# A three-stage fp32 kernel on one core: sums of squares added by transfers, the last downward products of a tile placed behind the next tile's second pair

## The chip, the core and the metric

The kernel runs on one core of a Trainium2 chip. The metric is the time of one execution on the device, in microseconds (us); the median of three runs before the change is 1011.33 us.

## What is computed

```python
mag = np.sqrt(a_re * a_re + a_im * a_im)
scale = np.minimum(mag, 0.999) / (mag + 1e-06)
a_re_n, a_im_n = (a_re * scale, a_im * scale)
for t in range(S):                       # B, H, S, D = 4, 8, 768, 48
    ar, ai = (a_re_n[:, :, t, :, None], a_im_n[:, :, t, :, None])
    new_re = ar * S_re - ai * S_im
    new_im = ar * S_im + ai * S_re
    kv = np.einsum('bhd,bhe->bhde', k[:, :, t], v[:, :, t])
    S_re, S_im = (new_re + kv, new_im)
    y[:, :, t] = np.einsum('bhd,bhde->bhe', q[:, :, t], S_re)
# then, with x = y as (3072, 384):
h = x @ w_in                             # d_ff 2048
x = (np.maximum(h, 0.0) + np.log1p(np.exp(-np.abs(h)))) @ w_out
h = (x @ w1) * (x @ w2) @ w3             # d_ff 1024
out = h @ w_out2
```

## The kernel before, in words

The 3072 tokens are eight tiles of 384. A tile passes three stages. The **preparation** (ScalarE, VectorE) makes from `a_re`, `a_im`, `q`, `k` the decayed queries and keys: it normalizes a by its magnitude, multiplies the a of eight neighbouring tokens up (`run` 1 to 7), combines the ends of these runs (`ends`, `carry` 1 to 32), multiplies the carries in (`by`, `p`), makes `tt` = q p (`q`) and `pp` = k / p (`inverse`, `keys`, `keys end`). Two sums of squares stand in it, both of two halves of the tile `te`, 128 x 1152 each: |a|^2 (`m2`) ahead of the square root, and |p|^2 (`p2`) ahead of the reciprocal. ScalarE squares both halves, VectorE adds them (L928 and L1017), ScalarE takes the logarithm (L663 and L692) and exponentials, and VectorE refines with Newton steps (`newton`, `scale start`, `scale`, `a`; or `inverse`). `tt` and `pp` go to memory and come back with another layout (`stq`, `stk`).

The **attention** of a tile is six groups (`scores` L1317 and L1320, mask on VectorE L1119, `outputs` L1340 to L1349). ScalarE copies each group's y to `ys` (L721), and small transfers place it into `x1raw` (`store_y`, L416, eight per chunk of 128 tokens, issued by SyncE). The **first network** takes `x1raw` split in two halves of precision (`x1h`, `x1l`), in eight pairs of 128 columns: `up` (18 products into `ps_ay` for pair 0 and into `ps_p` for the others), the softplus on ScalarE (Abs L732, Exp L736, Ln L738) and VectorE (`add_relu`, L1165), the split `g_h` (ScalarE, L745) and `g_l` (VectorE, L1172), and `down` (18 products into `ps_2`). At the end of a tile `x2_out` (ScalarE, L787) copies `ps_2` over `x1raw`, which SyncE stores. The second network runs after the eighth tile.

The order is written out by hand for each engine, in a function `slot(n, ...)` of eight steps j. Slot n holds the first network of tile n, the attention of tile n + 1, the preparation of tile n + 2 and the first sum of tile n + 3. On TensorE step j is `up` of pair j + 1, the scores of group j, `down` of pair j, the outputs of group j. In step 6 `up` of the next tile's pair 0 follows, and step 7 is `down` of pair 7. On VectorE the dictionaries `before_mask`, `after_mask` and `after_sum` tell which pieces of the preparation stand where in a step. Each engine waits for semaphores in its own order: SyncE's transfers and ScalarE's and VectorE's instructions behind a wait stand still with it. `up` of a pair above 0 waits for the `add_relu` of the pair before it, the scores of group 0 for the `add_relu` of the running tile's pair 0, since both use `ps_ay`. GpSimd computes only in the second network (`ab_low`).

Before the first slot come the preparations of tiles 0 and 1 and the attention of tile 0, one after the other, while the weights are loaded and split.

## Time and profile before

| | |
|---|---|
| runs | 1012.21, 1008.62, 1011.33 us, median 1011.33 |
| profiled execution | 1010.65 us, span 1008.9 us |
| busy in the span | PE 912.0 us (90%), DVE 607.4 (60%), ACT 426.8 (42%), POOL 70.4 (7%) |
| mean granted TensorE clock | 0.959 |

PE is TensorE, PEld its weight loads, DVE VectorE, ACT ScalarE, POOL GpSimd, SP SyncE. A share of busy time is a mean over the start, the seven tile slots, and the second network; the stretches and waits of the section after the next tell them apart. "Idle before" is the time for which an engine stood still ahead of an instruction, with what released it. Neighbouring matmuls overlap, so the durations of the single ones add up to more than the time they take.

### The profile page before, as it was taken

The numbers are of one execution on the slowest core, as the hardware profiler recorded it, in microseconds if no ns is written. First come the engines' busy times: TensorE is split into PE (matmuls) and PEld (weight loads), VectorE is DVE, ScalarE is ACT, GpSimd is POOL, SyncE is SP. The second block draws the span as 40 slices with busy tenths as digits, with TensorE's granted clock in tenths as the row PEclk, the third lists the DMA queues.
The fourth block names the chain that finished last, engine by engine and source line by source line (L and its number), as shares of the span: only waits on it lengthen the run. The fifth ranks groups of instructions, "written<-read, shape, count | busy, mean of one in ns | idle before, by whom it ended". The sixth has DMA issues, their size and how long they took to land.

```text
span 1008.9 us, 14507 instructions
## 1 busy us (share of the span) xinstructions
PE 912.0 (90%) x5442; PEld 828.5 (82%) x5442; DVE 607.4 (60%) x966; ACT 426.8 (42%) x618; POOL 70.4 (7%) x56
## 2 busy tenths in 40 slices
PE   0964839999999999999989999987999999999998
PEld 0533739988999888989889999987888888888887
DVE  5977978989989989989899723445121212121211
ACT  3152254673764664853854654667011111212011
POOL 0000000000000000000000000000222222222221
PEclk9985569999999999999999999999999999999999
DMA  9676074381470570560650630232101010101000
GB/s 338 227 201 176 20 205 110 106 196 55 137 207 13 152 192 10 169 176 13 196 145 12 174 78 12 72 124 79 32 1 63 1 63 0 62 0 63 1 32 32
DMA packets 98663, 99.52 MB, mean 99 GB/s; under 512 B 6944, under 2 KB 91936, under 8 KB 98592
## 3 DMA queue, kind: packets, MB, share of 16 engines
q1 hardware_dynamic: 98592, 98.59, 34.1%
q8 instruction: 42, 0.69, 0.3%
q14 instruction: 29, 0.24, 0.1%
HBM read 63.96 MB, written 29.88 MB: 93 GB/s over the span
## 4 chain that ended last, share of the span: by engine, by line
PE 47%; DVE 28%; DVEq 9%; ACT 8%; issue 4%; DMA 3%; ACTq 1%; SPq 0%
PE ps_p L1281 5%; PE ps_p L1282 5%; PE ps_p L1283 5%; DVE sp L1165 4%; DVEq L921 3%; PE ps L1469 3%; PE ps L1467 3%; PE ps L1468 3%; DVE g_l L1172 2%; DVE am L1119 2%; PE ps L1281 2%; PE ps L1283 2%; PE ps L1282 2%; PE ps_ay L1317 2%; DVE an L953 2%
## 5 line engine op out<-in xcount | busy, mean ns | idle before, releaser
L1281 PE MATMUL ps<-g_h,wo_h 128*128 128x384 f32 x384 | 133.5, 348 | 7.1 <-DVE g_l L1172 7.1
L629 POOL TENSOR_TENSOR abl<-ab,abh 128x512 fp32r<-128x512 f32 x48 | 69.5, 1447 | 931.7 <-DVE abh L1263 931.7
L1281 PE MATMUL ps_p<-x1h,win_h 128*128 128x384 f32 x336 | 117.3, 349 | 15.7 <-DVE sp L1165 15.3
L1283 PE MATMUL ps<-g_h,wo_l 128*128 128x384 f32 x384 | 129.4, 337 | 0.0
L1282 PE MATMUL ps<-g_l,wo_h 128*128 128x384 f32 x384 | 129.1, 336 | 0.0
L1283 PE MATMUL ps_p<-x1h,win_l 128*128 128x384 f32 x336 | 113.1, 337 | 0.0
L1282 PE MATMUL ps_p<-x1l,win_h 128*128 128x384 f32 x336 | 113.0, 336 | 0.0
L745 ACT ACTIVATE g_h<-sp 128x768 fp32r<-128x768 f32 (+1 forms) x71 | 55.5, 781 | 98.2 <-DVE sp L1165 98.2
L1317 PE MATMUL ps_ay<-stq,stk 96*128 96x128 f32 x384 | 57.5, 298 | 34.7 <-DMA vt<-in_v 13.3
L1254 DVE TENSOR_TENSOR ab<-ps_ay,bc 128x512 f32<-128x512 f32 x24 | 16.6, 693 | 117.0 <-ACT bc L892 117.0
L1317 PEld LDWEIGHTS ps_ay<-stq,stk 96*128 96x128 f32 x384 | 54.9, 211 | 35.9 <-issue 23.4
L1254 DVE TENSOR_TENSOR ab<-ps_p,bc 128x512 f32<-128x512 f32 x24 | 16.6, 693 | 110.4 <-ACT bc L892 110.4
L732 ACT ACTIVATE sp<-ps_p 128x768 f32<-128x768 f32 (+1 forms) x63 | 46.3, 736 | 81.2 <-PE ps_p L1283 81.2
L1281 PEld LDWEIGHTS ps<-g_h,wo_h 128*128 128x128 f32 x384 | 72.7, 189 | 9.5 <-DVE g_l L1172 9.4
L1281 PEld LDWEIGHTS ps_p<-x1h,win_h 128*128 128x128 f32 x336 | 63.6, 189 | 19.7 <-DVE sp L1165 19.0
L1165 DVE SCALAR_TENSOR_TENSOR sp<-ps_p,sp 128x768 f32<-128x768 f32 (+1 forms) x63 | 54.6, 867 | 39.0 <-ACT sp L738 35.5
L1172 DVE TENSOR_TENSOR g_l<-sp,g_h 128x768 fp32r<-128x768 f32 (+1 forms) x71 | 62.3, 878 | 24.4 <-ACT g_h L745 19.0
L1282 PEld LDWEIGHTS ps<-g_l,wo_h 128*128 128x128 f32 x384 | 72.8, 190 | 0.0
L1283 PEld LDWEIGHTS ps<-g_h,wo_l 128*128 128x128 f32 x384 | 72.5, 189 | 0.0
L892 ACT ACTIVATE bc<-ps_p 128x512 f32<-128x512 f32 x24 | 14.4, 599 | 126.4 <-PE ps_p L1283 126.4
L892 ACT ACTIVATE bc<-ps_k 128x512 f32<-128x512 f32 x24 | 14.4, 599 | 126.0 <-PE ps_k L1283 126.0
L1282 PEld LDWEIGHTS ps_p<-x1l,win_h 128*128 128x128 f32 x336 | 63.7, 190 | 0.0
(147 smaller groups left out, 2053.4 us busy)
## 6 DMA issues: line engine op xcount, KB each, us to landing
qk_scr<-tt SPq DMA_DIRECT2D x16, 576.0 KB, 4.5
stq<-qk_scr SPq DMA_DIRECT2D x48, 192.0 KB, 4.8
qk_scr<-pp SPq DMA_DIRECT2D x16, 576.0 KB, 4.1
stk<-qk_scr SPq DMA_DIRECT2D x48, 192.0 KB, 4.6
an<-in_a_re SPq DMA_DIRECT2D x8, 576.0 KB, 4.1
an<-in_a_im SPq DMA_DIRECT2D x8, 576.0 KB, 5.2
qk<-in_q SPq DMA_DIRECT2D x8, 576.0 KB, 7.5
qk<-in_k SPq DMA_DIRECT2D x8, 576.0 KB, 8.7
```

The costliest lines, as they stand in the source:

```text
L629: tensor_tensor(abl[:, m % AR, :], ab[:, m % 2, :], abh[:, m % AR, :].bitcast(F32), ALU.subtract).then_inc(ab_lo, 1)
L732: act(buf, ps_u[j][:, us, 0:T], ACT.Abs)
L745: act(g_h[:, j % GR, us, :], sp[:, j % 2, us, :], ACT.Copy).then_inc(g_hi, us.stop - us.start)
L921: eng.drain()
L1165: ve.scalar_tensor_tensor(out=buf, in0=ps_u[j][:, us, 0:T], scalar=0.0, in1=buf, op0=ALU.max, op1=ALU.add)\
L1172: ve.tensor_tensor(g_l[:, j % GR, us, :], sp[:, j % 2, us, :], g_h[:, j % GR, us, :].bitcast(F32), ALU.subtract).then_inc(g_lo, us.stop - ...
L1254: ve.tensor_tensor(ab[:, m % 2, :], ps_ab[m % 2][0], bc[:, m % 2, :], ALU.mult).then_inc(ab_mul, 1)
L1281: mm(o, wh, xh, start=start, stop=False)
L1282: mm(o, wh, xl, start=False, stop=False)
L1283: return mm(o, wl, xh, start=False, stop=stop)
L1317: last = mm(ps_a[:, h4, :], stk[0:D2, h, cs], stq[0:D2, h, cs], start=True, stop=True)
L1467: mm(ps_o[s_], ah, w34h[:, m, :], start=m == 0, stop=False)
```

## The change

1. The two adds of squares leave VectorE. GpSimd issues a transfer from one half of `te` to the other that adds (`accum_op`), 16 in all, and ScalarE's logarithm waits for its landing.
2. The transfers of y (`store_y`) move from SyncE's queue to GpSimd's. There `sum_psquares` of a tile stands behind the y of group 3, and `sum_squares` behind that of group 4 and ahead of that of group 5.
3. On TensorE `down` of a tile's pair 7 moves behind `up` of the next tile's pair 1; each part of `down` of pair 0 waits for its own third of `x2_out`.
4. ScalarE: `x2_out` moves between Abs and the rest of pair 1's softplus; the logarithm of |a|^2 moves from ahead of `x1_high` to between Abs and Exp of pair 7; both squares of p come between Abs and Exp.
5. VectorE: `scale` moves ahead of `add_relu` of pair 0, and `a` is split in two, the first half ahead of `g_low`; `run` 7, `by` and later pieces are spread anew, `keys end` goes to step 6.

The diff, without the hunks that only pass a new argument and that on VectorE ahead of the first slot:

```diff
@@ -467,10 +460,6 @@
             wait(w34_ev, NM2)
             eng.dma_start(w34_scr.rearrange("c p n -> p c n"), w34s[:, :, :]).then_inc(w34_wr, 16)
             load_piece(7)
-
-            wait(raw_lo, 5)
-            for i in range(NG):
-                store_y(0, i)
             wait(prep_p, 4)
             load_a(2)
             store_q(1)
...
@@ -486,29 +475,17 @@
 
                 if not first:
                     store_x2(n - 1)
-                if att:
-
-                    if first:
-                        wait(x1_lo, 2)
-                    else:
-                        x2_landed(n - 1)
-                    for i in range(NG - 2):
-                        store_y(n + 1, i)
                 if prep:
                     wait(prep_p, 2 * n + 6)
                     if nxt:
                         load_a(n + 3)
                     store_q(n + 2)
-                if att:
-                    store_y(n + 1, NG - 2)
                 if prep:
 
                     wait(yz_mm, NG * n + NG + 4)
                     for c in range(2):
                         stack_q(n + 2, c)
                         load_v(n + 2, c)
-                if att:
-                    store_y(n + 1, NG - 1)
                 if prep:
                     store_k(n + 2)
                     for c in range(2):
...
@@ -629,6 +606,45 @@
                 tensor_tensor(abl[:, m % AR, :], ab[:, m % 2, :], abh[:, m % AR, :].bitcast(F32),
                               ALU.subtract).then_inc(ab_lo, 1)
 
+            def store_y(m, i):
+                c, hq = i // 2, i % 2
+                eng.wait_ge(y_ev, NG * m + i + 1)
+                for u, row, rows, pairs, p0, gs_ in Y_MOVES[hq]:
+                    eng.dma_start(x1raw[p0:p0 + rows, gs_, CT * c:CT * c + CT], ys[64 * u + row:64 * u + row + rows, i % 2, pairs, :])\
+                        .then_inc(y_wr[i], 16)
+
+
+            def sum_squares(m):
+                eng.wait_ge(prep_sq, m + 1)
+                eng.dma_start(te[:, 0, :], te[:, 1, :], accum_op=ALU.add).then_inc(prep_m2, 16)
+
+            def sum_psquares(m):
+                eng.wait_ge(prep_psq, m + 1)
+                eng.dma_start(te[:, 0, :], te[:, 1, :], accum_op=ALU.add).then_inc(prep_p2, 16)
+
+            sum_squares(0)
+            sum_psquares(0)
+            sum_squares(1)
+
+            eng.wait_ge(raw_lo, 5)
+            for i in range(NG):
+                store_y(0, i)
+            sum_psquares(1)
+            sum_squares(2)
+            for m in range(1, NT):
+
+                if m == 1:
+                    eng.wait_ge(x1_lo, 2)
+                else:
+                    for mo in range(G):
+                        eng.wait_ge(x2_wr[mo], 16 * m)
+                for i in range(NG):
+                    store_y(m, i)
+                    if m < NT - 1 and i == 3:
+                        sum_psquares(m + 1)
+                    if m < NT - 2 and i == 4:
+                        sum_squares(m + 2)
+
             with eng.Fori(0, NT2) as t:
                 for m in range(NM2):
                     ab_low(t, m)
...
@@ -659,7 +675,7 @@
                 last.then_inc(prep_sq, 1)
 
             def prep_log(m):
-                eng.wait_ge(prep_m2, m + 1)
+                eng.wait_ge(prep_m2, 16 * m + 16)
                 act(te[:, 1, :], te[:, 0, :], ACT.Ln)
 
             def prep_root(m):
...
@@ -730,7 +746,7 @@
                     buf = sp[:, j % 2, us, :]
                     eng.wait_ge(p_mm, after(n, j, us))
                     act(buf, ps_u[j][:, us, 0:T], ACT.Abs)
-                    if between is not None:
+                    if between is not None and us.start == 0:
                         between()
                     eng.drain()
                     act(buf, buf, ACT.Exp, scale=-1.0)
...
@@ -808,25 +824,27 @@
                     if j < NP1 - 2:
 
                         def between():
+                            if prev and j == 0:
+
+                                eng.wait_ge(x1_lo, 2 * n + 2)
+                                x2_out(n - 1)
                             if has_prep and j == 4:
-                                prep_psquare(n + 2, 0)
-                            k_by_tokens(n + 1, j)
-
-                        softplus(n, j + 1, split, between if att else None)
-                        if has_prep and j == 4:
-                            prep_psquare(n + 2, 1)
+                                prep_psquares(n + 2)
+                            if att:
+                                k_by_tokens(n + 1, j)
+
+                        softplus(n, j + 1, split, between)
                         if nxt_prep and j == 5:
                             prep_squares(n + 3)
                         g_high(n, j + 1, split)
                     elif j == NP1 - 2:
-                        if nxt_prep:
-                            prep_log(n + 3)
-                            prep_root(n + 3)
                         if nxt:
                             for part in range(2):
                                 y_loaded(n + 1, part)
                                 x1_high(n + 1, part)
-                        softplus(n, j + 1, split)
+                        softplus(n, j + 1, split, (lambda: prep_log(n + 3)) if nxt_prep else None)
+                        if nxt_prep:
+                            prep_root(n + 3)
                         g_high(n, j + 1, split)
                         if nxt_prep:
                             prep_root_square(n + 3)
...
@@ -837,13 +855,10 @@
                         w2_high(j)
                     elif weights and j == 2 * G:
                         w34_high()
-
-                if nxt:
-                    eng.wait_ge(x1_lo, 2 * n + 4)
-                if not weights:
+                if not nxt and not weights:
                     x2_out(n)
 
-            slot(0, True, True, True)
+            slot(0, True, True, True, prev=False)
             for n in range(1, NT - 3):
                 slot(n, True, True, True)
             slot(NT - 3, True, True, False)
...
@@ -924,9 +939,7 @@
                 eng.drain()
 
             def prep_m2_(m):
-                eng.wait_ge(prep_sq, m + 1)
-                ve.tensor_tensor(te[:, 0, :], te[:, 0, :], te[:, 1, :], ALU.add).then_inc(prep_m2, 1)
-                eng.drain()
+                pass
 
             def prep_newton(m):
 
...
@@ -949,9 +962,8 @@
                                         op0=ALU.add, op1=ALU.mult)
                 eng.drain()
 
-            def prep_a(m):
-                ve.scalar_tensor_tensor(out=an[:, :, :], in0=an[:, :, :], scalar=-1e-6,
-                                        in1=tr[:, :].unsqueeze(1).to_broadcast([P, 2, GT]), op0=ALU.mult, op1=ALU.mult)
+            def prep_a(m, c):
+                ve.scalar_tensor_tensor(out=an[:, c, :], in0=an[:, c, :], scalar=-1e-6, in1=tr[:, :], op0=ALU.mult, op1=ALU.mult)
                 eng.drain()
 
             def prep_run(i):
...
@@ -1075,10 +1085,10 @@
             by = [("by", c, part) for part in range(2) for c in range(2)]
 
 
-            before_mask = {0: ["scale", "a"], 1: steps("run", 3, 4, 5), 2: ["ends"] + steps("carry", 1, 2),
-                           3: steps("carry", 16, 32) + by[:2], 4: ["p"], 5: ["inverse"]}
-            after_mask = {0: steps("run", 1), 1: steps("run", 6), 2: steps("carry", 4), 3: by[2:3], 4: ["q"], 5: ["keys"]}
-            after_sum = {0: steps("run", 2), 1: steps("run", 7), 2: steps("carry", 8), 3: by[3:], 4: ["p2"], 5: []}
+            before_mask = {0: steps("a", 1), 1: steps("run", 3, 4), 2: steps("run", 7) + ["ends"] + steps("carry", 1),
+                           3: steps("carry", 8, 16, 32), 4: by[3:] + ["p"], 5: ["p2", "inverse"]}
+            after_mask = {0: steps("run", 1), 1: steps("run", 5), 2: steps("carry", 2), 3: by[:2], 4: ["q"], 5: []}
+            after_sum = {0: steps("run", 2), 1: steps("run", 6), 2: steps("carry", 4), 3: by[2:3], 4: [], 5: ["keys"]}
 
             def raw_low(i):
 
...
@@ -1189,11 +1198,15 @@
                         mask_scores(n + 1, j)
                     if has_prep and j < 6:
                         prep(n + 2, even, after_mask[j])
+                    if has_prep and j == 6:
+                        prep(n + 2, even, ["keys end"])
                     if j == 6 and nxt:
                         x1_low(n + 1)
                     if j < NP1 - 1:
                         add_relu(n, j + 1, split)
                     elif nxt:
+                        if nxt_prep:
+                            prep(n + 3, not even, ["scale"])
                         add_relu(n + 1, 0, False)
                     if has_prep and j < 6:
                         prep(n + 2, even, after_sum[j])
...
@@ -1201,13 +1214,11 @@
                         prep(n + 3, not even, ["m2"])
                     if j < NP1 - 1:
                         g_low(n, j + 1, split)
-                        if has_prep and j == 5:
-                            prep(n + 2, even, ["keys end"])
                         if nxt_prep and j == 6:
-                            prep(n + 3, not even, ["newton"])
+                            prep(n + 3, not even, ["newton", "scale start"])
                     elif nxt:
                         if nxt_prep:
-                            prep(n + 3, not even, ["scale start"])
+                            prep(n + 3, not even, steps("a", 0))
                         g_low(n + 1, 0, False)
                     if weights and j == 1:
                         eng.wait_ge(ok_cnt, 1)
...
@@ -1375,8 +1386,6 @@
 
             def down(n, j, split):
 
-                if j == 0:
-                    eng.wait_ge(x2_ev, G * n + G)
                 if split:
                     order = [(mo, u) for u in range(2) for mo in range(G)]
                 else:
...
@@ -1385,6 +1394,9 @@
                 for mo, u in order:
                     if split and mo == 0:
                         eng.wait_ge(g_lo, after(n, j, slice(0, u + 1)) + 4)
+
+                    if j == 0 and u == 0:
+                        eng.wait_ge(x2_ev, G * n + mo + 1)
                     ms_ = slice(P * mo, P * (mo + 1))
                     c = 2 * j + u
                     last = mm3(ps_2[:, mo, 0:T], wo_h[:, c, ms_], wo_l[:, c, ms_], g_h[:, j % GR, u, :],
...
@@ -1400,14 +1412,17 @@
                 eng.wait_ge(s_new, states(NT, 0))
                 mm(ps_k[0:1, 0:1], stats[:, 5 * NT:5 * NT + 1], ones[:, 0:1], start=True, stop=True).then_inc(ok_cnt, 1)
 
-            def slot(n, att, even, nxt=True, flag_after=None):
+            def slot(n, att, even, nxt=True, prev=True, flag_after=None):
 
                 for j in range(NP1):
                     if j < NP1 - 1:
                         up(n, j + 1)
+                    if prev and j == 0:
+                        down(n - 1, NP1 - 1, False)
                     if att and j < NG:
                         scores(n + 1, j)
-                    down(n, j, not att)
+                    if not nxt or j < NP1 - 1:
+                        down(n, j, not att)
                     if att and j < NG:
                         outputs(n + 1, j, not even)
                     if nxt and j == NP1 - 2:
```

ScalarE from the copy of the last y of a tile (the row with `ys`) to the first pair of the next. Before:

```order
L721 ACTIVATE ys<-ps_ay 112x256
L663 ACTIVATE te<-te 128x1152
L667 ACTIVATE te<-te 128x1152
L702 ACTIVATE x1h<-x1raw 128x3x256
L702 ACTIVATE x1h<-x1raw 128x3x128
L732 ACTIVATE sp<-ps_p 128x768
L736 ACTIVATE sp<-sp 128x768
L738 ACTIVATE sp<-sp 128x768
L745 ACTIVATE g_h<-sp 128x768
L674 ACTIVATE tt<-te 128x1152
L732 ACTIVATE sp<-ps_ay 128x768
```

And after:

```order
L737 ACTIVATE ys<-ps_ay 112x256
L718 ACTIVATE x1h<-x1raw 128x3x256
L718 ACTIVATE x1h<-x1raw 128x3x128
L748 ACTIVATE sp<-ps_p 128x768
L679 ACTIVATE te<-te 128x1152
L752 ACTIVATE sp<-sp 128x768
L754 ACTIVATE sp<-sp 128x768
L683 ACTIVATE te<-te 128x1152
L761 ACTIVATE g_h<-sp 128x768
L690 ACTIVATE tt<-te 128x1152
L748 ACTIVATE sp<-ps_ay 128x768
```

The logarithm (L663, now L679) and the root (L667, now L683) moved behind the two parts of `x1h`, one before and one behind Exp and Ln.

VectorE behind the last pair's `g_l`, up to the mask of the next slot. Before:

```order
L1172 TENSOR_TENSOR g_l<-sp,g_h 128x768
L935 SCALAR_TENSOR_TENSOR tr<-te,tt 128x1152
L938 SCALAR_TENSOR_TENSOR te<-tr,te 128x1152
L1165 SCALAR_TENSOR_TENSOR sp<-ps_ay,sp 128x768
L944 TENSOR_SCALAR tr<-te 128x1152
L1172 TENSOR_TENSOR g_l<-sp,g_h 128x768
L948 SCALAR_TENSOR_TENSOR tr<-te,tr 128x1152
L953 SCALAR_TENSOR_TENSOR an<-an,tr 128x2304
L1119 TENSOR_TENSOR am<-ps_ay,mask 128x512
```

And after:

```order
L1182 TENSOR_TENSOR g_l<-sp,g_h 128x768
L948 SCALAR_TENSOR_TENSOR tr<-te,tt 128x1152
L951 SCALAR_TENSOR_TENSOR te<-tr,te 128x1152
L957 TENSOR_SCALAR tr<-te 128x1152
L961 SCALAR_TENSOR_TENSOR tr<-te,tr 128x1152
L1175 SCALAR_TENSOR_TENSOR sp<-ps_ay,sp 128x768
L966 SCALAR_TENSOR_TENSOR an<-an,tr 128x1152
L1182 TENSOR_TENSOR g_l<-sp,g_h 128x768
L966 SCALAR_TENSOR_TENSOR an<-an,tr 128x1152
L1129 TENSOR_TENSOR am<-ps_ay,mask 128x512
```

Ahead of the add that frees `ps_ay` (L1165, now L1175) two more passes stand, and half of `a` ahead of `g_l`.

GpSimd in one tile, where nothing stood before:

```order
L613 DMA x1raw<-ys 48x2x128 x2
L623 DMA te<-te 128x1152
L613 DMA x1raw<-ys 48x128 x2
L613 DMA x1raw<-ys 32x128
L613 DMA x1raw<-ys 16x128 x2
L613 DMA x1raw<-ys 32x128
L619 DMA te<-te 128x1152
L613 DMA x1raw<-ys 48x2x128 x2
```

The y of groups 3, 4 and 5, with the tile's second sum (L623) behind the first of them and the first sum of the next tile but one (L619) ahead of the last.

## Rows read from the trace of the kernel before

**Rows 1.** Busy time of each engine in the stretch of one tile (us, busy, instructions)

```profile
379.00:451.00 72.00, 69.42 (x496) 65.73 (x495) 63.78 (x101) 43.62 (x62) 0.00 (x0) 1.00 0.45 124
```

**Rows 2.** Who waited for whom: us in total, times, longest

```profile
PE ps_p L1281 <- DVE sp L1165: 15.3, 16, 3.1
...
PE ps_ay L1317 <- DMA vt<-in_v: 13.3, 1, 13.3
...
PE ps L1281 <- DVE g_l L1172: 7.1, 7, 1.2
```

**Rows 3.** Timeline of TensorE at a tile change: start, us, what, [idle before]

```profile
428.35 0.44 PE L1281 MATMUL ps_ay<-x1h,win_h 128*128 128x384 f32 x1
...
432.96 0.44 PE L1281 MATMUL ps<-g_h,wo_h 128*128 128x384 f32 x1 [1.20 <-DVE g_l L1172]
...
446.08 0.44 PE L1281 MATMUL ps_p<-x1h,win_h 128*128 128x384 f32 x1 [0.40 <-DVE sp L1165]
```

**Rows 4.** DMA issues: KB each, median us from issue to landing

```profile
qk_scr<-pp SPq DMA_DIRECT2D x16, 576.0 KB, 4.1
...
qk<-in_k SPq DMA_DIRECT2D x8, 576.0 KB, 8.7
...
x1raw<-ys SPq DMA_DIRECT2D x48, 48.0 KB, 2.0
```

**Rows 5.** Timeline of ScalarE at the start, squares and logarithms alone

```profile
8.06 1.15 ACT L658 ACTIVATE te<-an 128x1152 f32<-128x1152 f32 x1
...
10.72 1.16 ACT L663 ACTIVATE te<-te 128x1152 f32<-128x1152 f32 x1
...
52.88 2.43 ACT L682 ACTIVATE te<-pp 128x1152 f32<-128x1152 f32 x2 [16.57 <-DVE pp L1004]
...
58.14 1.16 ACT L692 ACTIVATE te<-te 128x1152 f32<-128x1152 f32 x1 [2.83 <-DVE te L1017]
...
64.71 1.15 ACT L658 ACTIVATE te<-an 128x1152 f32<-128x1152 f32 x1
...
68.84 1.16 ACT L663 ACTIVATE te<-te 128x1152 f32<-128x1152 f32 x1 [2.89 <-DVE te L928]
...
123.93 2.21 ACT L682 ACTIVATE te<-pp 128x1152 f32<-128x1152 f32 x2
...
129.63 1.16 ACT L692 ACTIVATE te<-te 128x1152 f32<-128x1152 f32 x1 [2.26 <-DVE te L1017]
```

**Rows 6.** Groups by line: VectorE's passes; busy us, mean ns

```profile
L953 DVE SCALAR_TENSOR_TENSOR an<-an,tr 128x2304 f32<-128x2304 f32 x8 | 20.5, 2559 | 0.6
...
L928 DVE TENSOR_TENSOR te<-te 128x1152 f32<-128x1152 f32 x8 | 10.8, 1350 | 6.9 <-ACT te L658 6.9
...
L944 DVE TENSOR_SCALAR tr<-te 128x1152 f32<-128x1152 f32 x8 | 6.0, 752 | 0.2
```

**Rows 7.** Timeline of ScalarE, then VectorE, at the same tile change

```profile
422.70 0.37 ACT L721 ACTIVATE ys<-ps_ay 112x256 f32<-112x256 f32 x1
...
426.77 0.53 ACT L702 ACTIVATE x1h<-x1raw 128x384 fp32r<-128x384 f32 x1 [0.16 <-DMA x1raw<-ys]
...
429.93 0.96 DVE L1165 SCALAR_TENSOR_TENSOR sp<-ps_p,sp 128x768 f32<-128x768 f32 x1 [1.64 <-ACT sp L738]
...
433.00 1.36 DVE L935 SCALAR_TENSOR_TENSOR tr<-te,tt 128x1152 f32<-128x1152 f32 x1
...
435.94 0.96 DVE L1165 SCALAR_TENSOR_TENSOR sp<-ps_ay,sp 128x768 f32<-128x768 f32 x1
```

**Rows 8.** Timeline of ScalarE around a tile's second sum

```profile
408.14 0.48 ACT L712 ACTIVATE kt<-ps_k 128x384 f32<-128x384 f32 x1
...
410.37 1.15 ACT L682 ACTIVATE te<-pp 128x1152 f32<-128x1152 f32 x1
...
413.36 1.17 ACT L692 ACTIVATE te<-te 128x1152 f32<-128x1152 f32 x1
```

**Rows 9.** One line's instructions (L416): ns least, median, most

```profile
L416 SPq DMA_DIRECT2D x1raw<-ys x192: 556/592/1636, 97.8 to 635.9; - x192
```

More of the change, by code:

```diff
@@ L410, in stack_k @@
                         .then_inc(k_rd[c], 16)
-            def store_y(m, i):
-                c, hq = i // 2, i % 2
-                wait(y_ev, NG * m + i + 1)
-                for u, row, rows, pairs, p0, gs_ in Y_MOVES[hq]:
-                    eng.dma_start(x1raw[p0:p0 + rows, gs_, CT * c:CT * c + CT], ys[64 * u + row:64 * u + row + rows, i % 2, pairs, :])\
-                        .then_inc(y_wr[i], 16)
             def load_x1(n, m):
@@ L1015, in prep_p2_ @@
             def prep_p2_(m):
-                eng.wait_ge(prep_psq, m + 1)
-                ve.tensor_tensor(te[:, 0, :], te[:, 0, :], te[:, 1, :], ALU.add).then_inc(prep_p2, 1)
-                eng.drain()
+                pass
             def prep_inv_newton(m):
@@ L1131, in _ @@
             raw_low(0)
-            prep(0, True, ["newton", "scale start", "scale", "a"] + steps("run", 1, 2))
+            prep(0, True, ["newton", "scale start", "scale"] + steps("a", 0, 1) + steps("run", 1, 2))
             raw_low(1)
@@ L1138, in _ @@
             prep(0, True, steps("carry", 8, 16, 32) + by + ["p", "q", "p2", "inverse", "keys", "keys end"], first=True)
-            prep(1, False, ["m2", "newton", "scale start", "scale", "a"])
+            prep(1, False, ["m2", "newton", "scale start", "scale"] + steps("a", 0, 1))
             for i in range(4, 7):
@@ L1175, in _ @@
             add_relu(0, 0, False)
-            prep(2, True, ["newton"])
+            prep(2, True, ["newton", "scale start", "scale"] + steps("a", 0))
             g_low(0, 0, False)
-            prep(2, True, ["scale start"])
             def slot(n, att, has_prep, nxt_prep, even, nxt=True, weights=False):
@@ L1418, in _ @@
             up(0, 0)
-            slot(0, True, True)
+            slot(0, True, True, prev=False)
             for n in range(1, NT - 3):
```

12 lines of the change are left out of this document (6 added, 6 removed).

## The prediction

> **What bounds the kernel now.** I read the stretches first, then who TensorE waits for, then the timelines at two places: the start, where the two first tiles are prepared, and the change from one tile to the next. In the stretch of one tile, TensorE is busy 69.42 of 72 us and VectorE 63.78 [rows 1]. So the seven tile changes and the steps between them are bound by TensorE, with VectorE close behind it. The waits say how close: over the whole program TensorE idles 15.3 us in 16 places for VectorE's `sp` (the softplus sum that frees `ps_p`) and 7.1 us in 7 places for `g_l` [rows 2]. These 22.4 us are all that a lighter VectorE can win in the tiles. The reader should see that the `g_l` waits come once per tile, all before the last pair's downward products (432.96, 1.20 us) [rows 3].
>
> The start is another regime. There the preparation of tile 0 and then of tile 1 is one chain over ScalarE and VectorE. After it TensorE waits 13.3 us in one place for a load of `vt` [rows 2], which SyncE issues only after the keys of tile 1 are stored. Anything put into that chain moves the whole rest of the program. Each sum of squares lies in it: ScalarE squares, VectorE adds, ScalarE takes the logarithm.
>
> **The change, part by part.** The one unknown price is L, the time from the end of the second square on ScalarE to the start of the logarithm when a transfer issued by GpSimd adds in between. No transfer that adds, and none of GpSimd's, is in this trace. The nearest row below is a 48 KB transfer between on-chip tiles, 2.0 us from issue to landing; the nearest of the same size, 576 KB, is the store of `pp`, 4.1 us; the slowest of that size is `qk<-in_k`, 8.7 us [rows 4]. A transfer that adds must also read what it adds to. Counting the moving part of the 4.1 us row (4.1 - 2.0 = 2.1) twice gives 6.2. I take L = 5.2, the middle of 4.1 and 6.2, with 3.1 (half way from 2.0 to 4.1) and 8.7 as ends.
>
> For this rows give only a bracket. The Trainium skill ("DMA: Bandwidth & Descriptors", Anatomy of one DMA, SWDGE path) fits a GpSimd transfer as 2.0 us plus bytes over 436 GB/s, 3.35 us for 589,824 bytes; by that estimate the sum below would end at +1.2 us instead of +15.2. This case's store row, 4.1 us, is slower than the fit; and another page ("Collectives: The Full Stack", Part 3) says that an adding transfer needs two source reads and runs at half the rate of a copy. No run here shows it yet.
>
> *The start.* Five sums lie in the chain. From end of the second square to logarithm the trace has: tile 0's first, 8.06 + 1.15 = 9.21 to 10.72, 1.5 us; its second, 55.31 to 58.14, 2.8 us (VectorE multiplied by `qk` first); tile 1's first, 65.86 to 68.84, 3.0 us; its second, 126.14 to 129.63, 3.5 us [rows 5]. Tile 2's first repeats the third, 3.0 us. Together 13.8 us, against 5 L. At L = 5.2 the start gets 26.0 - 13.8 = +12.2 us longer. The other work of VectorE there (a `raw` piece, `q`) already stands inside these gaps, so it hides nothing more. This is the largest term.
>
> *VectorE's relief.* Two adds of 1.35 us per tile leave it [rows 6], 2.7 us of some 64. TensorE's waits for `sp` are 15.3 us over six tiles that have preparation beside them, 2.5 per tile. The pieces are spread more evenly (`run 7` goes one step later, `ends` stays, `by` is split over steps 3 and 4), but the fourth step keeps `p` and `q`, and a product piece of 1.35 us more ahead of its mask, so I let only a third go: 0.8 us x 6 = -4.8 us.
>
> *The tile change.* The last downward products of tile n now stand behind tile n + 1's second upward pair. TensorE has two upward groups of 18 products (3.2 us each, 428.35 onwards [rows 3]) in front of them instead of one, so the wait for `g_l` goes. For the two last tile changes, which have no preparation, that is all: 7.1 / 7 = 1.0 us each [rows 2], -2.0 us. In the five with preparation something is late next. ScalarE's copy of `ys` ends at 422.70 + 0.37 = 423.07; the last part of `x1h` starts at 426.77, ended by the transfer of `ys` [rows 7]. Before, logarithm and root filled that time. Now the logarithm stands between Abs and Exp behind it, 1.17 us, and VectorE's add of the last pair ends at 430.9 + 1.2 = 432.1; the second upward group could start at 428.35 + 3.2 = 431.5 and waits 0.6. It ends at 435.3, the downward products at 438.5. VectorE meanwhile takes the two Newton steps (from 433.00, now from 434.3) and then, ahead of the next tile's first add, also `scale start` 0.75 and `scale`, 1.35 like every such pass over 1152 elements [rows 6]; so that add, which ended at 436.9 (435.94 + 0.96), ends at about 440.2. The next scores use the same bank and wait for it: 438.5 to 440.3. Behind it stands half of `a` (2.56 / 2 = 1.3 us) and `g_low`, 0.9: 442.5, for which the first downward products wait another 1.0. They and the outputs take 4.6: 447.1, where the trace has 446.08 [rows 3]. That is 1.0 us later, x 5 = +5.0 us. The copies of `x2` out, now after Abs of the second pair, lie beside these waits and cost nothing; without those waits they would delay Exp by 1.2 us.
>
> *The late second sum.* In a tile the second square ended at 410.37 + 1.15 = 411.52 and the logarithm began at 413.36, 1.84 us. Both squares now stand before `kt`, Exp and Ln, which took from 408.14 to 410.37, 2.2 us; so a sum has 1.8 + 2.2, some 4.1 us, before it stalls ScalarE [rows 8]. At L = 5.2 it is 1.1 us late. Behind the waiting logarithm are Abs of the next pair on ScalarE and, on VectorE, `inverse` and the mask of the last scores, for which TensorE's outputs wait. With 0.3 us of slack that is 0.8 x 6 = +4.8 us.
>
> *The moved transfers.* All 24 small transfers of a tile's y go from SyncE to GpSimd, which computes nothing in this part. SyncE gets free of them; no one waits for its other transfers inside the tiles, so that is worth nothing. On GpSimd the y of the last scores stands behind the first sum of the tile after next. The squares end 1.5 us before `ys` is written, so at L = 5.2 the sum lands 3.7 us after, when y landed in the trace as well: nothing, but a us per us beyond.
>
> The sum is 12.2 - 4.8 - 2.0 + 5.0 + 4.8 = +15.2 us. The profiled execution took 1010.65 us, 0.7 under the median of the runs, 1011.33; so 1026 us, 1.5% slower.
>
> **The rivals.**
> *Faster: VectorE's relief decides.* If TensorE loses all 7.1 us for `g_l` and two thirds of the 15.3 for `sp` (-17.3), and the tile change costs nothing, with L = 4.1 (start 20.5 - 13.8 = +6.7), the time is 1010.65 - 10.6 = 1000 us. For it speaks VectorE's share in the tiles. Against it speaks that the start pays first, and that `scale` ahead of the add is a chain by itself. It decides where the tiles win more than 5 L - 13.8. Chance 0.20.
> *No change: a cheap transfer.* With L = 3.1 the start costs 1.7, the second sum is in time, and 1.7 - 4.8 - 2.0 + 5.0 = -0.1 gives 1011 us. The skill's fit named above would give 1012. Against it stands the 4.1 us row. Chance 0.14.
> *Much slower: the adding transfer is slow.* With L = 8.7 the start costs 29.7, the second sum 4.3 x 6 = 26, and the y behind the first sum 3.5 x 5 = 17: together with the other terms 1082 us; half way from the forecast is 1054. The load during the first 20 us, when the weights come in, speaks for a large L at least once. Chance 0.15.
> *GpSimd's issuing is slow.* SyncE takes 0.59 us to issue a y transfer [rows 9]; if GpSimd needs 1.5, six of them fill a step, and first sums and last y come 2 us late: +12 more, 1038. Chance 0.07.
>
> **How the numbers follow.** My forecast has the remaining 0.44, between 1016 (L = 4.1: start +6.7, no late sum, +4.9 in all) and 1040. The range leaves out more than half of the faster case and of the very slow one: 1003 to 1050. About 0.5%, 5 us, is what a measurement tells from no change. Faster: 0.20; within 0.5%: 0.14; slower: 0.66.
>
> **What would show it.** Right: the transfer `te<-te` lands 4 to 6 us after its issue; the first mask of tile 0 comes some 8 us later than now, tile 1's scores 12; no wait for `g_l` before the last downward products, but one of 1 to 2 us at the next scores, released by VectorE's add; a ScalarE wait of a us for the transfer before the second logarithm, six times. Wrong: `te<-te` lands in under 3.5 us or over 7; the distance from a tile's second pair to the next tile's falls from some 72 us [rows 1] under 70; or ScalarE waits longest for the y transfer, not for the sum.

## The result, and the profile after

The changed kernel takes 1071.76 us (median of 6 runs, 1068.56 to 1074.72), the kernel before in the same session 1010.38 (1008.62 to 1012.61): ratio 1.060, interval 1.058 to 1.061. The direction was forecast, the size was not: 1026 us, with 1050 as the upper end. The profiled span grew from 1008.9 to 1066.8 us, by 57.9.

Where in the program did it go? Busy time by stretch; the boundaries are the passes that write `x1l` for a next tile, the same places in both kernels. First the kernel before (columns: stretch, length, busy us and instructions of PE, PEld, DVE, ACT, POOL, then granted clock, DMA share, GB/s):

```profile
0.00:127.00 127.00, 76.65 (x328) 54.18 (x328) 99.34 (x171) 40.72 (x54) 0.93 (x8) 0.79 0.61 192
127.00:210.00 83.00, 66.78 (x453) 63.72 (x454) 71.46 (x108) 45.88 (x62) 0.00 (x0) 0.87 0.55 143
210.00:282.00 72.00, 69.25 (x491) 65.89 (x490) 64.07 (x103) 44.25 (x65) 0.00 (x0) 1.00 0.47 124
282.00:354.50 72.50, 68.17 (x481) 64.35 (x480) 64.21 (x106) 42.67 (x60) 0.00 (x0) 1.00 0.45 123
354.50:427.00 72.50, 69.58 (x492) 66.10 (x491) 64.22 (x104) 44.26 (x64) 0.00 (x0) 1.00 0.44 123
427.00:499.30 72.30, 67.97 (x480) 64.22 (x479) 64.05 (x105) 42.78 (x60) 0.00 (x0) 1.00 0.46 124
499.30:571.30 72.00, 68.84 (x489) 65.52 (x488) 62.80 (x102) 39.59 (x58) 0.00 (x0) 1.00 0.41 108
```

The changed kernel, the same stretches:

```profile
0.00:144.00 144.00, 76.63 (x328) 53.87 (x328) 95.77 (x170) 40.47 (x53) 16.86 (x36) 0.77 0.61 187
144.00:240.00 96.00, 70.05 (x451) 66.90 (x452) 66.62 (x105) 43.64 (x59) 15.83 (x28) 0.81 0.58 143
240.00:319.20 79.20, 73.37 (x490) 69.63 (x490) 61.87 (x101) 44.38 (x65) 14.48 (x26) 0.94 0.51 131
319.20:397.30 78.10, 70.64 (x482) 67.41 (x481) 61.85 (x104) 42.97 (x59) 14.48 (x26) 0.96 0.48 121
397.30:475.80 78.50, 70.97 (x491) 67.08 (x489) 61.90 (x102) 44.03 (x63) 14.47 (x26) 0.98 0.50 132
475.80:554.60 78.80, 70.69 (x481) 67.35 (x481) 61.78 (x104) 43.14 (x59) 14.44 (x26) 0.96 0.49 126
554.60:629.50 74.90, 69.39 (x490) 65.49 (x489) 61.98 (x102) 41.90 (x60) 13.48 (x25) 1.00 0.44 112
```

The first two stretches give 17 + 13 = 30 us. The next four tiles give 7.2, 5.6, 6.0 and 6.5 us, the fifth 2.9. The sixth is even 0.8 us shorter (66.9 against 67.7), and from 696 us on (639 before) only 0.5 us is lost. So there are two effects, at the start and in the tiles. Look also at PE's busy column in the third stretch: 69.25 against 73.37 us for the same number of instructions but one. TensorE does not only wait longer, it runs slower; more on this below.

**The start.** ScalarE's timeline, the squares and logarithms of tile 0 and the second of tile 1 (start, us, [idle before]), where [rows 5] had 10.72, 58.14 and 129.63:

```profile
7.79 1.15 ACT L674 ACTIVATE te<-an 128x1152 f32<-128x1152 f32 x1
...
19.61 1.16 ACT L679 ACTIVATE te<-te 128x1152 f32<-128x1152 f32 x1 [9.21 <-DMA te<-te]
...
62.02 2.44 ACT L698 ACTIVATE te<-pp 128x1152 f32<-128x1152 f32 x2 [19.63 <-DVE pp L1016]
71.78 1.16 ACT L708 ACTIVATE te<-te 128x1152 f32<-128x1152 f32 x1 [7.32 <-DMA te<-te]
...
140.93 2.21 ACT L698 ACTIVATE te<-pp 128x1152 f32<-128x1152 f32 x2
151.71 1.16 ACT L708 ACTIVATE te<-te 128x1152 f32<-128x1152 f32 x1 [5.27 <-DMA te<-te]
```

From the end of the second square to the logarithm: 10.7, 7.3 and 8.6 us; tile 1's and tile 2's first sums take 5.5 and 5.6. The five together take 37.7 us, where before they took 13.8: +23.9. It reaches TensorE nearly whole: its first scores of tile 0 start at 92.39 instead of 77.21 us, those of tile 1 at 174.28 instead of 149.80, 24.5 later.

**The transfer.** DMA issues (KB each, median us from issue to landing), where [rows 4] had 4.1 for the store of `pp`:

```profile
te<-te POOLq DMA_DIRECT2D x16, 576.0 KB, 6.3
qk_scr<-tt SPq DMA_DIRECT2D x16, 576.0 KB, 7.0
...
qk_scr<-pp SPq DMA_DIRECT2D x16, 576.0 KB, 4.5
```

The adding transfer lands 5.0 to 10.2 us after its issue. The store of `tt` took 4.5 us in the kernel before and takes 7.0 now. Two runs told of below bear on that: with the same orders but the sums on VectorE the store takes 4.5 us again, and with all sums by transfers in the old orders 4.6. In the changed kernel SyncE issues it 1.8 us behind the adding transfer (454.85 and 456.61 us), in that other run 0.3 to 0.7 us ahead of it (384.50 and 384.76). So it is the adding transfer that slows the store in this order; that a store issued just ahead of it goes free fits these rows.

**The tiles.** Waits (total us, times, longest), of the changed kernel, beside [rows 2]:

```profile
ACT te L708 <- DMA te<-te: 29.7, 8, 7.3
...
ACT te L679 <- DMA te<-te: 17.6, 3, 9.2
...
PE ps_ay L1351 <- DVE am L1129: 16.0, 6, 3.6
...
PE ps_p L1292 <- DVE sp L1175: 12.9, 10, 3.1
...
PE ps_ay L1328 <- DVE sp L1175: 11.4, 5, 2.3
```

The first sum makes ScalarE wait at the start alone (3 times); in the tiles its logarithm stands late enough. The second is late in all six tiles that have one beside them, by 2.8 to 3.6 us in five and 1.1 in the last. One instance, from the timelines of POOL, ACT, DVE and PE in this order:

```profile
454.85 0.97 POOL L623 DMA_DIRECT2D te<-te  x1 [5.00 <-ACT te L698]
```
```profile
461.84 1.17 ACT L708 ACTIVATE te<-te 128x1152 f32<-128x1152 f32 x1 [2.79 <-DMA te<-te]
```
```profile
464.37 1.36 DVE L1033 TENSOR_TENSOR tr<-te 128x1152 f32<-128x1152 f32 x1 [4.28 <-ACT te L711]
...
467.26 0.69 DVE L1129 TENSOR_TENSOR am<-ps_ay,mask 128x512 f32<-128x512 f32 x1
```
```profile
468.10 0.43 PE L1351 MATMUL ps_ay<-stq,state 96*48 96x128 f32 x4 [2.45 <-DVE am L1129]
```

The squares end at 454.54, 0.3 us before GpSimd's issue, the logarithm starts at 461.84, `inverse` waits for the exponential, the mask waits behind `inverse` in VectorE's order, and TensorE's outputs wait for the mask.

**The clock.** What TensorE was granted right behind that wait (PE's granted clock is the third value from the end; 1.00 is 2.4 GHz and 0.50 is 1.2):

```profile
467.00:469.00 2.00, 0.90 (x16) 0.86 (x16) 1.91 (x4) 1.99 (x4) 0.00 (x0) 1.00 1.11 227
469.00:471.00 2.00, 2.00 (x17) 1.89 (x14) 1.58 (x2) 1.67 (x4) 0.83 (x1) 0.78 1.21 185
471.00:473.00 2.00, 2.00 (x8) 2.00 (x7) 2.00 (x3) 0.00 (x0) 1.29 (x3) 0.50 0.95 193
473.00:475.00 2.00, 2.00 (x12) 2.00 (x11) 1.19 (x1) 0.14 (x1) 0.00 (x0) 0.87 1.00 169
```

In the 2 us at 0.50 it executes 8 matmuls, in the next 2 us 12. TensorE had idled 1.25 us before 457.87 and 2.45 us before 468.10. Between 240 and 696 us the changed kernel has seven such drops; the kernel before has none in its tiles, its rows of 1 us from 215 to 640 all read 1.00. In the five tiles from 240 to 629.5 us PE's busy time is 4.1, 2.5, 1.4, 2.7 and 0.6 us larger than in the same tiles before, 11.3 us in all, with the program's matmuls unchanged. At the start it is 3.3 us larger (146.7 against 143.4 in the first two stretches). What follows the wait of 2.45 us costs (0.22 + 0.50 + 0.13) x 2 = 1.7 us more after it is over.

### The profile page after: what moved, and what is told of

It reads as the page before. It is cut to its first block, busy times and chain, and to the rows that moved or that the text cites. A ratio compares the mean times of both kernels' runs of the same rounds, so it can differ in the third digit from the quotient of the medians.

```text
span 1066.8 us, 14507 instructions
## 1 busy us (share of the span) xinstructions
PE 927.8 (87%) x5442; PEld 844.0 (79%) x5442; DVE 588.9 (55%) x958; ACT 427.5 (40%) x618; POOL 186.0 (17%) x264
## 4 chain that ended last, share of the span: by engine, by line
PE 53%; DVE 18%; DMA 10%; ACT 8%; DVEq 4%; issue 3%; ACTq 2%; POOL 0%; SPq 0%
DMA te<-te 7%; PE ps_p L1292 6%; PE ps_p L1293 6%; PE ps_p L1294 6%; PE ps L1292 3%; PE ps L1293 3%; PE ps L1294 3%; PE ps_ay L1328 3%; PE ps L1484 2%; PE ps L1482 2%; PE ps L1483 2%; PE ps_ay L1293 2%; PE ps_ay L1294 2%; DVE an L1009 2%; PE ps_ay L1292 2%
## 5 line engine op out<-in xcount | busy, mean ns | idle before, releaser
L613 POOL DMA_DIRECT2D x1raw<-ys x192 | 100.6, 532 | 418.4 <-ACT ys L737 410.2
L1292 PE MATMUL ps_p<-x1h,win_h 128*128 128x384 f32 x336 | 121.6, 362 | 12.9 <-DVE sp L1175 12.9
L1293 PE MATMUL ps_p<-x1l,win_h 128*128 128x384 f32 x336 | 117.0, 348 | 0.0
L1294 PE MATMUL ps_p<-x1h,win_l 128*128 128x384 f32 x336 | 116.8, 348 | 0.0
L1328 PE MATMUL ps_ay<-stq,stk 96*128 96x128 f32 x384 | 58.2, 300 | 63.9 <-DMA stk<-qk_scr 20.7
L1175 DVE SCALAR_TENSOR_TENSOR sp<-ps_p,sp 128x768 f32<-128x768 f32 (+1 forms) x63 | 54.6, 866 | 48.4 <-ACT sp L754 46.7
L1292 PEld LDWEIGHTS ps_p<-x1h,win_h 128*128 128x128 f32 x336 | 66.9, 199 | 16.6 <-DVE sp L1175 15.3
L1293 PEld LDWEIGHTS ps_p<-x1l,win_h 128*128 128x128 f32 x336 | 66.6, 198 | 0.0
L1294 PEld LDWEIGHTS ps_p<-x1h,win_l 128*128 128x128 f32 x336 | 66.5, 198 | 0.0
```

Source lines behind the costliest of these rows:

```text
L613: eng.dma_start(x1raw[p0:p0 + rows, gs_, CT * c:CT * c + CT], ys[64 * u + row:64 * u + row + rows, i % 2, pairs, :])\
L1175: ve.scalar_tensor_tensor(out=buf, in0=ps_u[j][:, us, 0:T], scalar=0.0, in1=buf, op0=ALU.max, op1=ALU.add)\
L1292: mm(o, wh, xh, start=start, stop=False)
L1293: mm(o, wh, xl, start=False, stop=False)
L1294: return mm(o, wl, xh, start=False, stop=stop)
L1328: last = mm(ps_a[:, h4, :], stk[0:D2, h, cs], stq[0:D2, h, cs], start=True, stop=True)
```

## The experiments

### The sums by themselves, and the orders by themselves

The changed kernel with both adds on VectorE again, the second ahead of `inverse` in step 5, the first ahead of `g_low`; orders, y on GpSimd and downward products as changed:

```
-            def prep_m2_(m):
-                pass
+            def prep_m2_(m):
+                eng.wait_ge(prep_sq, m + 1)
+                ve.tensor_tensor(te[:, 0, :], te[:, 0, :], te[:, 1, :], ALU.add).then_inc(prep_m2, 1)
...
```

> The changed kernel with both sums back on VectorE at the same places of its order, y still issued by GpSimd. Theory S (the late sums cost it): the five sums of the start took 37.7 us from squares to logarithm instead of 13.8, and in each slot the logarithm of the second sum waited some 3 us; without them 1071.8 - 24 - 6 x 3 = 1030 us or less, and if VectorE's chain at the tile change was late only because of them, 1010. Theory O (the new orders cost it, the sums only the start): 1071.8 - 24 = 1048 us, with the 2.3 us waits before the next slot's scores still there.

Measured 1036.28 us (1033.48 to 1042.62), 1.027 of before (1.024 to 1.031): between the 1030 of theory S and the 1048 of theory O, so each is half right. The sums by transfers are worth 35.5 us of the 61, and the orders cost 26 without them. VectorE's add in step 5 makes TensorE wait at the same place:

```profile
PE ps_ay L1345 <- DVE am L1123: 12.3, 6, 2.1
```

The reverse, the kernel before with all sums by transfers and nothing else:

```
+            sum_squares(0)
+            for m in range(NT):
+                sum_psquares(m)
+                if m < NT - 1:
+                    sum_squares(m + 1)
...
-                ve.tensor_tensor(te[:, 0, :], te[:, 0, :], te[:, 1, :], ALU.add).then_inc(prep_m2, 1)
...
```

> The kernel before with nothing but the sums issued by GpSimd, all orders old. Theory S: start +24 us; in a slot the old order leaves 1.8 us from the second squares to their logarithm and 1.6 us for the first, against 7 and 5.6: 5 x 6 + 4 x 5 = +50 us; 1080 to 1085. Theory O: the start's +24 and little more, since ScalarE has idle time: 1035 to 1045.

Measured 1094.3 us (1093.67 to 1094.57), 1.083: theory S's direction, 9 us above its band. ScalarE now waits for both sums in every tile, 88.3 us in all, where the changed kernel has 47.3:

```profile
ACT te L706 <- DMA te<-te: 52.0, 8, 8.3
ACT te L677 <- DMA te<-te: 36.3, 8, 9.4
PE ps_ay L1350 <- DVE am L1129: 35.0, 7, 7.0
```

So the rebuilt orders do what they are built for: given late sums they win 22.5 us (1094.3 to 1071.8). They pay for themselves only where the sums are late.

### The two small parts

y by SyncE again, as in the kernel before, the rest as changed:

```
+                    for i in range(NG - 2):
+                        store_y(n + 1, i)
...
```

> The changed kernel with the 192 y transfers back in SyncE's queue, sums still GpSimd's. If the y of the last group is late because it stands behind the first sum in GpSimd's queue, ScalarE's waits of 0.6 to 1.3 us for it go and the time falls by 3 to 6 us, to 1067. If the two share the DMA engines anyway: 1070 to 1073.

Measured 1069.17 us (1067.17 to 1070.71), 2.6 us less, with ranges that overlap. ScalarE's waits for y do not go, as the first branch had it; they are 8.5 us instead of 5.0. GpSimd's issue is no bottleneck. Issue times of one line in ns (least, median, most), first GpSimd's in the changed kernel, then SyncE's in this one:

```profile
L613 POOL DMA_DIRECT2D x1raw<-ys x192: 491/520/616, 114.7 to 693.5; - x192
```
```profile
L416 SPq DMA_DIRECT2D x1raw<-ys x192: 556/592/2171, 114.4 to 692.8; - x192
```

The kernel before with only the last pair's downward products and the copies of `x2` moved:

```
+                    if prev and j == 0:
+                        down(n - 1, NP1 - 1, False)
...
```

> The kernel before with the last downward products behind the next tile's second pair, and the copies of x2 moved with them, nothing else. If the waits for g_l (7.1 us in 7 places) go and nothing is late next: 1003 us. If ScalarE's copies of x2 between Abs and Exp delay the second pair's sum by as much: 1009 to 1012.

Measured 1008.8 us (1005.96 to 1012.07, 10 runs), 0.998 (0.9965 to 0.9996). That is near the second branch, but not by its cause. The 7.1 us of waits for `g_l` are gone, and 6.2 us come back at the outputs, for the masks, for which they waited 0.2 us before:

```profile
PE ps_ay L1346 <- DVE am L1122: 3.8, 3, 1.3
...
PE ps_ay L1343 <- DVE am L1122: 2.4, 3, 1.1
```

### Which order costs the 26 us

From here on the sums are on VectorE. The second sum goes from step 5 to step 4, where it was before:

```
-                           3: steps("carry", 8, 16, 32), 4: by[3:] + ["p"], 5: ["p2", "inverse"]}
+                           3: steps("carry", 8, 16, 32), 4: by[3:] + ["p"], 5: ["inverse"]}
...
-            after_sum = {0: steps("run", 2), 1: steps("run", 6), 2: steps("carry", 4), 3: by[2:3], 4: [], 5: ["keys"]}
+            after_sum = {0: steps("run", 2), 1: steps("run", 6), 2: steps("carry", 4), 3: by[2:3], 4: ["p2"], 5: ["keys"]}
```

> The changed kernel with both sums on VectorE as in e1b (1036 us), and the second sum's add moved back behind the add of step 4's pair instead of ahead of the Newton step in step 5. If the 2.0 us waits for the mask of the last scores, six of them in e1b, come from that place: they go and the time falls by 8 to 12 us, to 1026. If TensorE only waits for the same work one step earlier: 1034 to 1037.

Measured 1016.64 us (1015.38 to 1018.25), 1.005. This one piece, a pass of 1.35 us ahead of the last mask, six times, was 19.6 us of the 26, twice the 8 to 12 expected; the runs of the kernel with the pass in step 5 spread over 9 us, so the size is known to some 4 us either way. The two profiled executions lie 15.2 us apart, and there it adds up: the 12.3 us of waits at L1345 for the mask are gone, and TensorE is busy 3.1 us less (917.1 against 920.2).

Then also logarithm and root ahead of `x1h`, and `scale` behind the next tile's first add, as before:

```
+                        if nxt_prep:
+                            prep_log(n + 3)
+                            prep_root(n + 3)
                         if nxt:
...
-            before_mask = {0: steps("a", 1), 1: steps("run", 3, 4),
+            before_mask = {0: ["scale"] + steps("a", 0, 1), 1: steps("run", 3, 4),
```

> e1b with three places put back: the second sum's add in step 4, logarithm and root of the first sum ahead of the split of x1, and scale and a behind the next tile's first add. What is left of the change is the y on GpSimd, the moved downward products, and the spread of run, carry, by and keys end. If these three places are all that the new orders cost: 1036 - 26 = 1010, or, with the 2 us that the moved products win, 1008. If the spread costs by itself (the heavier step 3 and 4): 1015 to 1025. If the spread helps: under 1005.

Measured 1019.07 us (1016.69 to 1019.48), 1.0075 (1.006 to 1.009): nothing won, and inside the band for a spread that costs by itself. The 8.9 us that the scores waited for the add are gone, and in their place the outputs wait 7.2 us for the mask and the upward products 14.5 instead of 9.9 us for `sp`. Work of VectorE there can stand ahead of the add or of the mask; TensorE waits for it in either place.

Last the spread of `run`, `carry`, `by` and `keys` as before too:

```
-            before_mask = {0: ["scale"] + steps("a", 0, 1), 1: steps("run", 3, 4), 2: steps("run", 7) + ["ends"] + steps("carry", 1),
+            before_mask = {0: ["scale"] + steps("a", 0, 1), 1: steps("run", 3, 4, 5), 2: ["ends"] + steps("carry", 1, 2),
...
```

> The changed kernel with both sums on VectorE, and now the second sum, logarithm and scale, and also the spread of run, carry, by and keys as before; what is left of the change is y by GpSimd, both second squares ahead of kt's Exp, the copies of x2, and the downward products moved. Measured without the last step: 1019.1. Theory (the spread cost the rest, by a heavier step four): falls by 5 to 8 to 1011 to 1014. Rival (the spread is harmless, y or the squares' place cost it): stays at 1017 to 1020.

Measured 1015.6 us (1014.39 to 1017.33), 1.0036: 3.5 less, between the theory's band and the rival's, and the ranges of the two runs overlap. The spread cost about a third of the 10.3 us that were left. Of the 6.8 us that remain to the kernel with only the downward products moved, 2.3 are at the start, where the first upward group waits 7.3 us for `x1l` instead of 5.0, with y on GpSimd; the rest wasn't taken apart.

### The start alone, and the adding alone

The five sums of the start on VectorE, the other eleven by transfers:

```
-                eng.wait_ge(prep_m2, 16 * m + 16)
+                eng.wait_ge(prep_m2v, m + 1) if m < 3 else eng.wait_ge(prep_m2, 16 * m - 32)
...
```

> The changed kernel with the five sums ahead of the first slot on VectorE, the eleven others still by transfers. The start's sums took 37.7 us against 13.8: 1071.8 - 24 = 1048 us. If the start's delay were partly absorbed later (the tiles' own waits): 1053 or more.

Measured 1049.99 us (1045.86 to 1051.44), 1.037: 21.8 us less, against +23.9 read from the five gaps. Where it lies shows in the trace: the `x1l` pass that ends the first two stretches starts at 218.92 us, where it stood at 240.11 in the changed kernel and at 210.04 before. Behind it the six tiles take 462.0 us, 5.7 more than in the changed kernel, with more of the drops of the clock. So most of what stays is in the tiles, and a little of what the start wins is lost there.

A plain copy in place of the adding transfer. The sum of two halves is left out (ScalarE squares the first half twice), so that sizes and waits stay and only the addition goes:

```
-                eng.dma_start(te[:, 0, :], te[:, 1, :], accum_op=ALU.add).then_inc(prep_m2, 16)
+                eng.dma_start(te[:, 0, :], te[:, 1, :]).then_inc(prep_m2, 16)
...
```

> The changed kernel with a plain copy in the place of each adding transfer. ScalarE squares the first half twice, so that the copied values are of the right size; the sum itself is left out. If the add costs (a second read): te<-te lands in 4 to 4.5 us instead of 5.6 and 7.1 and the time falls by 5 x 1.5 in the start and 6 x 1.5 to 2.5 in the slots, to 1050 to 1056. If the other transfers on the same DMA engines cost: 5 us and more again, 1066 to 1072.

Measured 1043.32 us (1040.31 to 1052.86), 1.035, below the 1050 to 1056 expected: the adding itself costs 28 us over 16 transfers. Part of it comes by the waits that it lengthens: TensorE waits 8.5 us for masks instead of 16.0, and is busy 915.8 us instead of 927.8. The copy's landing, then the issue times of the copy and of the adding transfer of the changed kernel:

```profile
te<-te POOLq DMA_DIRECT2D x16, 576.0 KB, 4.9
```
```profile
L619 POOL DMA_DIRECT2D te<-te x8: 528/562/695, 9.3 to 526.3; - x8
L623 POOL DMA_DIRECT2D te<-te x8: 554/581/590, 62.0 to 587.8; - x8
```
```profile
L619 POOL DMA_DIRECT2D te<-te x8: 860/924/1055, 9.4 to 549.7; - x8
L623 POOL DMA_DIRECT2D te<-te x8: 888/964/970, 64.8 to 611.8; - x8
```

An addition adds 0.4 us of issue on GpSimd and 1.4 us to the median landing. The Trainium skill ("Collectives: The Full Stack", Part 3) has ReduceScatter, whose adding step reads two sources, at half the rate of AllGather, which copies. On one core, 6.3 against 4.9 us agree in the direction, the whole time being far from doubled. Even a copy would have made the kernel slower.

### A sum by a transfer where there is room

If the start and the second sum are what costs, the first sum of tiles 3 to 7 alone might win. On the kernel with the downward products moved (1008.8 us), with the logarithm in its old place:

```
+            for m in range(3, NT):
+                sum_squares(m)
...
```

> Kernel before with the last pair's downward products moved (1008.8 us when measured) and, in addition, only the first sum of tiles 3 to 7 by an adding transfer; the start's sums and all second sums stay on VectorE. The logarithm stays ahead of x1h. Theory (what decides is whether someone waits for the transfer): the logarithm starts 4 to 5 us after the second square in the old order, the transfer takes 6 to 7, so ScalarE waits 1 to 3 us per tile ahead of x1h, five times, and the second upward group of the next tile comes later: +2 to +8, 1011 to 1017. Rival (VectorE's relief of 1.35 us in five tiles is worth its face): -3 to -7, 1002 to 1006.

Measured 1037.83 us (1037.16 to 1038.38), 1.026: 29 us slower, far past both. The expectation had the room wrong: in that order only 2.0 us lie between second square and logarithm (square until 348.74, logarithm at 350.78), not 4 to 5. ScalarE waits 5.1 us per tile, and TensorE for `x1l` behind it:

```profile
PE ps_ay L1294 <- DVE x1l L1104: 28.7, 6, 5.2
...
ACT te L671 <- DMA te<-te: 25.7, 5, 5.5
```

And with the logarithm in its new place, behind Abs:

```
-                        if nxt_prep:
-                            prep_log(n + 3)
-                            prep_root(n + 3)
...
+                        softplus(n, j + 1, split, (lambda: prep_log(n + 3)) if nxt_prep else None)
```

> As the run before it, but logarithm and root stand behind Abs of the next tile's second pair, as in the changed kernel, where ScalarE never waited for this sum inside a tile. Theory: no wait for the transfer, VectorE relieved of 1.35 us in five tiles; the waits for sp fall a little: 0 to -4 against the kernel with only the downward products moved, 1005 to 1009. Rival (the later logarithm makes Newton and scale late, and the mask of the next scores with them): +3 to +6, 1012 to 1015.

Measured 1025.24 us (1025.12 to 1028.27), 1.014, 16 us slower. Nobody waits for the sum now. The rival's Newton steps are not it either: the outputs wait 6.4 us for masks, 6.2 without the transfer. ScalarE waits for another transfer:

```profile
DVE x1l L1103 <- ACT x1h L710: 13.0, 7, 3.6
PE ps_ay L1293 <- DVE x1l L1103: 11.6, 6, 5.0
ACT x1h L710 <- DMA x1raw<-ys: 11.6, 5, 2.6
```

The last y of a tile is issued while the sum is under way, and ScalarE waits 11.6 us in 5 places for it, where the kernel without the transfer does not wait. Neither theory had this. In one tile `ys` is written at 358.10 and the second part of `x1h` starts at 363.80, 5.7 us later; in the kernel before these were 423.07 and 426.77, 3.7 us [rows 7]. The adding transfer, issued at 356.56 after the squares end at 356.12, is under way in these us. That it slows the y transfer, as it did the store of `tt`, fits these rows; no run moved the one away from the other, so it is argued and not shown. TensorE's clock isn't it: PE is busy 912.9 us, as before.

## Why the prediction failed

The places were mostly right and the sizes too small; the price L was taken too low, and the clock was missing.

- **The price L.** "I take L = 5.2" is the step that failed first. Measured are 10.7, 7.3, 5.5, 8.6 and 5.6 us at the start, and in the tiles 7.3 to 7.8 in five and 5.6 in the sixth. The row of 4.1 us was a store; counting its moving part twice gave 6.2 as the upper of two middle values, and that is about what the transfer takes (6.3). Taking the middle with a plain store was the mistake. GpSimd's way to the issue (0.3) comes on top of the landing. The worst, 10.7, is the first, among the weights; that was said of the "much slower" rival, which took L = 8.7 and 1054 to 1082 us. It was given 0.15 and holds the result, in part by luck: its start of 29.7 was 23.9, its second sums of 26 were 16.0, its 17 for y were 5.0 us of ScalarE's waits, and it had no term for the clock. Fit and sum by the Trainium skill ("DMA: Bandwidth & Descriptors", Anatomy of one DMA), 3.35 us, are further off: even the copy's median was 4.9.
- **The start**, forecast +12.2: the five gaps give +23.9, the two first stretches +30. The mechanism (five sums in one chain) is confirmed by the run with those five on VectorE, -21.8. What the stretches have beyond the gaps is about the first late mask (3.1) and the slower TensorE (3.3).
- **VectorE's relief**, forecast -4.8: the waits for `sp` fell from 15.3 [rows 2] to 12.9, 2.4 us. The forecast laid all 15.3 on the tiles with preparation; 3.1 of them are one wait at 664.21 us, behind the last preparation, and it stayed.
- **`g_l`**, as forecast: gone. The waits that take their place, the scores for the next tile's first add, were forecast at 1.8 us and are 2.3 (11.4 in 5). The copies of `x2`, forecast at nothing, make TensorE wait 1.5. The run with only this part won 2 of 7.1 us, since the masks became late.
- **The late second sum**, forecast +4.8: the room of 4.1 us was read about right (4.5: 7.3 less the 2.8 of waiting), but with 7.3 instead of 5.2 the masks keep TensorE waiting 2.5 to 3.6 us in five tiles, 16.0 in all. That slack was none at all is seen with the sum on VectorE: 1.35 us ahead of the mask, six times, cost 19.6 us.
- **The clock** stood in no term. Every long wait of TensorE in the tiles was priced at its own length. Seven times the granted clock fell behind it from 1.00 to 0.50 for 3 to 7 us, +11.3 us of busy time. The Trainium skill ("TensorE: Matmul & The Clock Gate", HAM oscillation — how this bites in real kernels) tells of a kernel whose clock falls again and again behind waits for transfers; the rows here show the same behind waits for VectorE.

Put together, with the waits of TensorE in the six tiles alone (210 to 639 us before, 240 to 696.4 now): the start +30; in the tiles `sp` 11.0 to 8.3, `g_l` 6.3 to 0, scores 0 to 11.4, masks 0.2 to 12.9, copies of `x2` 0 to 1.5, `x1l` 0 to 0.3, together +16.9; busy time +11.3. The sum is 58.2, against 57.9 of the spans. This is bookkeeping over rows of two traces, not a test of each term; tested by runs are the start (21.8), the adding (28), the sums as a whole (35.5) and the second sum's place (19.6), which overlap and may not be added.

That GpSimd's issuing would be slow (0.07) and that VectorE's relief would decide (0.20) are both refuted. The second falls by the run in which nobody waits for a sum and VectorE has 1.35 us less in five tiles: it is 16 us slower, and TensorE's waits for `sp` rose there from 15.0 to 17.9.

## What to carry to other kernels

Before a vector pass of 1.35 us is given to a transfer, count the us from its operands' last write to its first reader in the order as it stands: here it needs 7, and the places had 2 and 4. Then look at which other transfers that someone waits for fall into these 7 us, since they can get slower as well. And a pass of an engine that isn't the bound can cost more than its length, here some 3 us for 1.35, if it stands ahead of the one thing that the bound engine waits for next; the order of the pieces, not the busy share (55% for VectorE), decides. A wait of TensorE can also cost more than it lasts, if its clock falls right afterwards.

## What the runs showed of the hardware

- An adding transfer of 576 KB between on-chip tiles, issued by GpSimd, lands 5.0 to 10.2 us after its issue (median 6.3) and takes 0.92 to 0.96 us to issue; as a copy 3.1 to 7.6 (median 4.9) and 0.56 to 0.58 us.
- GpSimd issues the small y transfers in 0.52 us, SyncE in 0.59.
- A store of the same size, issued 1.8 us behind it, goes from 4.5 to 7.0 us (6.0 behind the copy), and in the last experiment ScalarE waited 2.3 us per tile for y, which came 2.0 us later after `ys` than before.
- TensorE's clock fell to its lower level behind waits of 2.3 to 3.6 us in the changed kernel's tiles, seven times, but not behind every one: it stayed at 1.00 behind the idle 2.31 us before 412.57 and 2.27 us before 569.67. With the second sum early on VectorE (1016.64 us) it fell also behind shorter waits, 1.97, 1.91, 1.60 and 1.57 us (before 226.20, 300.23, 373.50 and 520.15); behind the last, TensorE was busy 0.61 and 0.79 us of the us from 521 and from 522, and then the clock fell. In the tiles of the kernel before, whose longest wait is 1.2 us, it never fell. In the kernel with only the first sums by transfer it fell in each of five tiles, behind waits of 4.0 to 5.2 us.
